# Group 0 of the mixing stage: tile 0's product ahead of the last input pieces of group 1, and one test for an empty pass of GpSimd's tile loop

## What is computed

```python
def _moe_ref(x, mu_k, mu_r, w_k, w_v, w_r):
    x_prev = shift(x, 1)                       # the token before, zeros ahead of the first
    xk = mu_k * x + (1.0 - mu_k) * x_prev
    xr = mu_r * x + (1.0 - mu_r) * x_prev
    k = np.maximum(xk @ w_k, 0.0)
    v = k * k @ w_v
    r = 1.0 / (1.0 + np.exp(-(xr @ w_r)))
    return r * v

# then, for each token: logits and a local gate choose an expert e
    h = np.maximum(x[b, s] @ w1[e], 0.0)
    out[b, s] = p[e] * (h @ w2[e])
```

## Time and profile before

| | |
|---|---|
| median of 3 runs | 623.83 us (622.97 to 624.48) |
| the profiled execution, its own time | 623.96 us |
| its span, first to last instruction | 622.0 us |
| granted TensorE clock, mean | 0.998 of full speed |
| busy: TensorE matmul, weight load | 607.4 us, 504.2 us |
| busy: VectorE, ScalarE, GpSimd | 410.7 us, 321.4 us, 178.0 us |

### The profile page before, as it was taken

One profiled execution on the slowest core, in us unless ns is written; L12 is line 12 of the kernel. 1 busy time (PEld: TensorE's weight loads), 2 busy tenths in 40 slices (PEclk: granted clock), 3 DMA queues, 4 the chain that ended last, 5 costly groups with the idle time before them and its releaser, 6 DMA issues.

```text
span 622.0 us, 14718 instructions
## 1 busy us (share of the span) xinstructions
PE 607.4 (98%) x4483; PEld 504.2 (81%) x4484; DVE 410.7 (66%) x1164; ACT 321.4 (52%) x698; POOL 178.0 (29%) x241
## 2 busy tenths in 40 slices
PE   7999999999999999999999999999999999999996
PEld 6878888888788888889979878788788888888884
DVE  3767779745779697786879958957736235463531
ACT  5767779677515714641643844647526125362531
POOL 4545545600000000000000331585732521553141
PEclk9999999999999999999999999999999999999999
DMA  8987886002210010001004661886933512764000
GB/s 303 377 282 243 274 286 205 18 2 85 66 71 0 1 51 18 0 21 48 0 18 170 222 250 46 284 312 206 343 127 121 204 58 94 239 223 133 12 17 15
DMA packets 32935, 84.66 MB, mean 136 GB/s; under 512 B 4602, under 2 KB 7418, under 8 KB 32896
## 3 DMA queue, kind: packets, MB, share of 16 engines
q1 hardware_dynamic: 26816, 70.03, 32.4%
q0 software_dynamic: 3200, 8.92, 4.2%
q10 hardware_dynamic: 2880, 5.24, 2.7%
HBM read 76.04 MB, written 9.70 MB: 138 GB/s over the span
## 4 chain that ended last, share of the span: by engine, by line
PE 86%; DVE 8%; issue 2%; ACT 2%; DMA 1%; SPq 0%; POOL 0%; DVEq 0%; ACTq 0%; POOLq 0%
PE banks L885 22%; PE banks L887 22%; PE banks L886 22%; PE banks L756 3%; PE banks L1075 3%; PE banks L823 2%; DVE we_lo L1527 2%; PE banks L832 2%; PE banks L786 2%; PE banks L770 1%; PE banks L994 1%; DMA vw<-in_v_t 1%; PE banks L800 1%; PE banks L796 1%; PE banks L847 1%
## 5 line engine op out<-in xcount | busy, mean ns | idle before, releaser
L1494 DVE CUSTOM_DVE_ANT_0 product<-x,xT 128x512 f32<-128x512 f32 x120 | 77.9, 688 | 0.5 <-DMA xT<-in_w 0.4
L1791 ACT ACTIVATE prob<-neg,negmax 128x160 f32<-128x160 f32 (+1 forms) x136 | 59.1, 436 | 29.4 <-DVE negmax L1205 19.7
L1769 DVE TENSOR_SCALAR hid<-banks 128x512 f32<-128x512 f32 x34 | 23.5, 691 | 72.8 <-PE banks L887 71.7
L1901 ACT ACTIVATE k_sum<-banks 128x512 f32<-128x512 f32 (+2 forms) x40 | 21.4, 534 | 90.9 <-PE banks L887 86.3
L885 PE MATMUL banks<-we_hi,hid_hi 128*128 (+1 forms) x160 | 66.6, 416 | 0.2 <-DVE hid_lo L1602 0.2
L885 PE MATMUL banks<-we_hi,xg_hi 128*128 (+1 forms) x160 | 64.7, 404 | 0.9 <-DVE we_lo L1527 0.9
L686 POOL MEMSET xg<- 128x1024 f32 x1 | 1.0, 957 | 220.9 <-ACT k_raw L1894 220.9
L887 PE MATMUL banks<-we_hi,hid_lo 128*128 (+1 forms) x160 | 62.7, 392 | 0.0
L887 PE MATMUL banks<-we_hi,xg_lo 128*128 (+1 forms) x160 | 62.6, 391 | 0.0
L886 PE MATMUL banks<-we_lo,hid_hi 128*128 (+1 forms) x160 | 62.5, 391 | 0.0
L886 PE MATMUL banks<-we_lo,xg_hi 128*128 (+1 forms) x160 | 62.4, 390 | 0.0
(11 more groups left out here) (295 smaller groups left out, 1470.1 us busy)
## 6 DMA issues: line engine op xcount, KB each, us to landing
xT<-in_w_e SPq DMA_DIRECT2D x36, 512.0 KB, 5.1
raw_end<-in_w_e SPq DMA_DIRECT2D x36, 512.0 KB, 5.0
qk<-in_qk_t SPq DMA_DIRECT2D x32, 448.0 KB, 6.3
vw<-in_v_t SPq DMA_DIRECT2D x32, 256.0 KB, 5.2
w_raw<-in_w_mix ACTq DMA_DIRECT2D x20, 256.0 KB, 4.2
x_rows<-x SPq DMA_DIRECT2D x17, 256.0 KB, 2.0
xT<-in_w SPq DMA_DIRECT2D x8, 256.0 KB, 3.3
vz<-in_v_z SPq DMA_DIRECT2D x8, 128.0 KB, 3.4
```

Source lines behind the costliest of these rows:

```text
L1494: dve.tensor_tensor_reduce(product[:, k % 2, :], x2[:, t, :], w9(e), 1.0, 0.0, ALU.mult, ALU.add, dot[:, t % 2, e:e + 1]).then_inc(dotted, 1)
L1769: dve.tensor_scalar(hid[:, D * h:D * (h + 1)], ps_h[:, h, :], 0.0, None, ALU.max).then_inc(hid_ready, 1)
L1791: act.activation(prob[:, t % 2, c], neg[:, c], ACT.Exp, scale=-1.0, bias=negmax[:, t % 2, k:k + 1], accum_out=rsum[:, t % 2, k:k + 1]).the ...
L1901: act.activation(k_sum[:, f % 2, 0:w], ps_k[:, f % 2, 0:w], ACT.Relu).then_inc(k_copied, 1)
```

## The change

On VectorE, in group 0 alone, `mix_inputs(1, 1, ...)` is cut after its first two pieces. The other three steps now come after the product of tile 0 (line 1554) and ahead of tile 0's dot products. Nothing is added or left out, and the other groups keep their order. ScalarE's and TensorE's programs are as before.

On GpSimd, the second tile of a pass is tested inside the test of the first: a pass whose first tile doesn't exist makes one test in place of two.

```diff
             with pool.Fori(1, MT // 2) as k:
-                for b, i in ((1, 2 * k + 1), (0, 2 * k + 2)):
-                    with pool.If(i < tiles):
-                        ...
+                def tile(i, b):
+                    ...
+                with pool.If(2 * k + 1 < tiles):
+                    tile(2 * k + 1, 1)
+                    with pool.If(2 * k + 2 < tiles):
+                        tile(2 * k + 2, 0)
...
+                elif first_group(g):
+                    mix_inputs(g + 1, 0, tiles_after)
+                    mix_inputs(g + 1, 1, tiles_after, range(0, 2))
                 else:
                     mix_inputs(g + 1, 0, tiles_after)
                     mix_inputs(g + 1, 1, tiles_after)
...
                     dve.tensor_tensor(x2[:, t, :], ps_v[:, parity(n0, t), :], x2[:, t, :], ALU.mult).then_inc(x2_ready, 1)
                     q0, q1 = sum(FILL[tiles][:t]), sum(FILL[tiles][:t + 1])
+                    if first_group(g) and t == 0:
+                        mix_inputs(g + 1, 1, tiles_after, range(2, DC + 1))
```

More of the change, by code:

```diff
@@ L713, in _ @@
             with pool.Fori(1, MT // 2) as k:
-                for b, i in ((1, 2 * k + 1), (0, 2 * k + 2)):
-                    with pool.If(i < tiles):
[L716 to L729, removed]
+                def tile(i, b):
+                    after = pool.value_load(table[0:1, bass.ds(MT + i, 1)], min_val=0, max_val=E)
+                    pool.wait_ge(xg_turned, i + 1)
+                    pool.sem_inc(stepped, 1)
+                    with pool.If(i + 2 < tiles):
+                        gather(i + 2, b, TOK)
+                    with pool.If(after > 0):
+                        last_parts(after, bass.ds(after % 2, 1))
+                    pool.drain()
+                    pool.wait_ge(y_stored[b], 16 * (k + 1 - b))
+                    pool.sem_inc(stepped, 1)
+                    scatter(i, b)
+                with pool.If(2 * k + 1 < tiles):
+                    tile(2 * k + 1, 1)
+                    with pool.If(2 * k + 2 < tiles):
+                        tile(2 * k + 2, 0)
             for b in range(2):
```

## The result

| | before | changed |
|---|---|---|
| median | 623.61 us (622.97 to 624.57, 11 runs) | 621.19 us (620.02 to 623.00, 11 runs) |
| profiled execution: own time, span | 623.96, 622.0 us | 623.00, 621.2 us |
| granted TensorE clock | 0.998 | 0.998 |

The ratio is 0.9961 with a 95% interval of 0.9951 to 0.9972: 2.4 us less. The profiled execution happens to be the slowest of the eleven, so its span fell by 0.8 us only. Where the rest went is the most instructive part of this case. I cut the span at four matmuls that can be found in every profile: the first key matmul of the mix, the first of group 1, the first expert matmul (`we_hi`, `xg_hi`), and the last one of all. Times are differences of the starts of TensorE's rows; the tail runs from the last matmul's start to the end of the span.

A forecast was written before the change was run, and what follows sets the result against it. TensorE bounds the kernel, with matmuls filling 98% of the span; GpSimd's loop ends it. From the profiled 623.96, minus 1.58 and 0.7, gives 621.7 us, a median of 621.5; eight-in-ten range 620.9 to 623.0 us.

The forecast's parts named there:

- Standing still and restart: TensorE ahead of tile 2's value sums in group 0: 1.42 us idle plus 0.16 us restarting, 1.58 us saved.
- The product is free in its new place: VectorE, group 0: tile 0's 0.69 us product fits a 0.89 us idle time, costing the pieces behind it nothing.
- What is late next: VectorE, group 0: tile 1's product ends about 171.5, 1.0 us before TensorE starts tile 3 at 172.46.
- cover: VectorE's idle time ahead of group 1's first rest of squares: 1.74 us of 3.32 us should remain.
- SyncE's store 0.5 us earlier: Tile 0's rows go out at about 168.1, not 168.57, sharing DMA engines with four loads; taken to cost nothing.
- Carried to the end: From group 1 on, all follows TensorE's progress, so 1.58 us lasts to the end; bounds 0 and 1.9 us.
- The loop: GpSimd at the program's end: three empty passes each save a 0.23 us test, 0.7 us; bounds 0 and 0.8.
- Rival (a): Program's end: the last scatter completes only at about 621.2, hiding the tail's gain; 622.3 us, chance 0.17.
- (b): After group 0: a later wait that doesn't move with TensorE swallows the first part; 623.1 us, chance 0.07.
- (c): Whole kernel: tail hidden and stall returning, so nothing measurable changes; 623.8 us, chance 0.06.
- (d): GpSimd's three empty passes: a longer jump needs a code fetch each time, making it slower; 628.1 us, chance 0.05.
- Rival (e): Behind group 0: ScalarE or VectorE waits also close up, or tests cost more; about 620.9 us, chance 0.08.

The follow-up runs named there:

- e1: The changed kernel with GpSimd's loop put back as before, so only VectorE's new order remains: median 622.00 us, ratio 0.9970 to before.
- e5: The changed kernel, but tile 0's product comes after four of the five steps of group 1's gate inputs, not two: median 622.23 us, ratio 0.9977 to before.
- e6: The changed kernel, but tile 0's product comes ahead of all five steps of group 1's gate inputs: median 625.09 us, ratio 1.0016 to before.

## Why the prediction was right, point by point

The forecast was 2.3 us less, from 623.83 to 621.5 us; the medians say 2.4 us, from 623.61 to 621.19, and the two stages of the profiles 2.3 us. Its terms, one by one:

- **Standing still and restart, 1.58 us.** Measured 1.57 in the first profile and 1.59 in e1: right, and in between as well, as e5 shows (0.62 us of standing still cost 56.79 - 56.01 = 0.78 us). The size of the restart, 0.16 us, was right; that it belongs to a stop was not, as the last section shows. Nothing in the sum hung on that.
- **The product is free in its new place.** The sums were there, the product started at 161.94 in the time of before (161.88 forecast), and piece 2 slipped by 0.02 us. Right.
- **What is late next.** Tile 1's product would have been late had the pieces slipped (e6); 1.1 us of margin for the 1.0 worked out. Idle time for the loads 1.17 us (1.1 forecast), cover 1.83 us (1.74 forecast). Right.
- **SyncE's store 0.5 us earlier.** Wrong in size: it was issued at 168.74, that is 168.45 in the time of before, 0.12 us earlier. From the end of its last load's issue (166.60 + 1.75 = 168.35) to the store SyncE took 0.39 us, which I had left out. It cost nothing, as taken.
- **Carried to the end.** Right in every kernel: 181.7 to 181.8 us between group 1 and the experts.
- **The loop.** 0.25 us a pass for 0.23, 0.75 us in all. Right. The step behind it was only just right: I put the scatter's completion near its last packet, 620.4, and it is 2.3 us after the scatter's start, 620.7 in the time of before. The forecast gain of 0.7 us came whole because this limit begins at 0.73, and that was luck: the reason given for it, a completion near the last packet, was wrong by 0.3 us. Rival (a) had the right mechanism with too late a completion.
- **Rivals (b), (c) and (d).** No later wait took the stall's place, and an empty pass takes 0.60 us, so no fetch stands behind the longer jump. The Trainium skill's rule on taken branches (Runtime: NRT & Kernel Launch, Instruction fetch mechanics) didn't come into play here; no run shows such a stall. Rival (e) needed other waits of group 0 to close up as well, and the stage gave 1.57 to 1.59 us and no more.
- **The spread.** The forecast compared one profile with one profile. Attention's end alone moves by over a microsecond between executions, and the accident adds 1.2 us; the median of 11 runs was needed to see 2.4 us.

## What to carry to other kernels

When the first group of a pipeline stalls and the others don't, look for what only it contains, here a table load. Then look for an idle time of the blocking engine into which the blocking instruction fits: it must be late enough for its operands and early enough for the one behind it, and both sides can be read off the trace. At the end of a program, compare the arrival at the last wait with the landing of the last transfer; work on the loop pays until the two meet. Compare stages between two landmarks, not whole spans, before blaming a change for a microsecond.

## What was not expected of the hardware

- A subtraction of 128x1024 values on VectorE that starts together with one on GpSimd and gets through second lasts 3.4 to 3.5 us, not 1.22; if it gets through first, GpSimd's lasts 3.43 us, not 2.40. Less than 0.1 us lies between the two starts, and the order is worth 1.2 us to TensorE.
- The last indirect scatter, which moved 0.05 MB, lands 2.3 us after its start on GpSimd, and only 0.3 to 0.4 us of that lie behind its last bytes.
- Behind the first matmul after a stop of 0.6 or 2.0 us the next one starts 0.33 us later, not 0.23 us (e5, e6), although the granted clock stays at 1.00. It isn't the stop: in group 1 of the kernel before TensorE didn't stop (222.79 to 223.01), and the step behind that matmul, to 223.35, is 0.34 us too. What the places have in common is the weight load. It was held back for the product, and starts together with its matmul and not one step ahead of it. The change leaves this in group 1 (221.73 to 222.06, 0.33 us), where the product still comes only just in time. The weight loads (PEld) at both places in the kernel before:

```profile
168.44 0.19 PEld L885 LDWEIGHTS banks<-wv_hi,k_hi 128*128 128x128 f32 x1 [1.69 <-DVE x L1554]
...
223.01 0.19 PEld L885 LDWEIGHTS banks<-wv_hi,k_hi 128*128 128x128 f32 x1 [0.26 <-DVE x L1554]
```
